# Reordering ScalarE's and VectorE's work in the last round before the final product, and moving one load ahead of stores

## The chip, the cores and the metric

The kernel runs on one core of one Trainium2 chip. The metric is the device time of one execution in microseconds (us); lower is better. Times shown beside each other come from runs of the same kernel on the same chip.

## What is computed

Attention with a window of 64 over 4 x 576 tokens and 8 heads of 64, then two feed-forward parts. Only the second one matters here:

```python
def _moe2_ref(x, w_in, w_out):          # x: 2304 x 512
    h = x @ w_in                        # 2304 x 2048
    g = np.maximum(0.01 * h, h)
    return (g @ w_out).astype(np.float32)
```

## The kernel before, in words

**Precision.** Every fp32 operand of a large product is split in two parts, hi (rounded to fp32r) and lo (the rest). ScalarE writes hi (an ACTIVATE Copy), VectorE then writes lo (a subtraction that reads hi). A product is three matmuls (`three_passes`, lines 387 to 391): hi x hi, hi x lo, lo x hi. Data are thus ready for TensorE only when VectorE's lo is written.

**Seven products for eight.** A block product is made by a Strassen-Winograd scheme: seven products P1 to P7 instead of eight, at the price of sums of the operands (g's sums here) and of the results (c11, c12, c21, c22). In the order of the code the products of a round are P1, P5, P6, P2, P7, P3, P4. ScalarE copies P1, P5 and P6 out of PSUM (`copy_p1`, `copy_p5`, `copy_u2`); VectorE adds P2, P7, P3 to them (`make_c11`, `make_c22`, `make_c12`).

**First product of the last part (x @ w_in).** 12 rounds, r = 15 to 26 (`h = r - HR0` = 0 to 11; HR = 12, OR0 = 27). A round is 14 half products of 6 matmuls of 128x384. After it ScalarE applies the leaky maximum in place: `leaky(r, 0)` to c11, `leaky(r, 2)` to c22, `leaky(r, 1)` to c12, and `leaky_c21` from PSUM. VectorE makes the sums of g: `g_sums13`, `g_sum2`, `g_sum4` for each of two halves s. SyncE stores the seven blocks of g to memory in four groups (`store_g(r, 0)` to `store_g(r, 3)`, of 1, 1, 3 and 2 DMAs of 384 KB each). The last round's g is not stored: it stays in SBUF and is used from there ("held").

**Second product (g @ w_out).** It runs over 84 parts k (`T_SEQ`), each of 12 matmuls. Each part of g is loaded back by `load_t(k)` on SyncE's queue (384 KB, DMA), unless held (k = 6, 7, 8, 12, ...), and split by `split_t(k)`, hi on ScalarE and lo on VectorE. `second_product(k)` waits for `t_lo >= k + 1`. The order of the first parts is P1's 0, 1, 2 (k = 0, 1, 2), P5's 0, 1, 2 (k = 3, 4, 5), then the held last parts of P1 and P5 (k = 6, 7), then P6 (k = 8 to 11). When part 6 is done, P1 is complete and `copy_p1(27)` may run; part 8 writes the same PSUM bank and waits for that copy (`bank_waits`, P6). On ScalarE `copy_p1(27)` stands behind `split_t(13)`, and so behind `split_t(11)` and `split_t(12)`.

**Buffers of the loads.** `t_raw` has 8 places. Parts 0 to 5, 9 and 10 take places 0 and 1 in turn; so `load_t(2)` waits for `t_lo >= 1`, `load_t(3)` for 2, `load_t(4)` for 3, `load_t(5)` for 4. Part 11 takes place 2 and part 13 place 3, which lie in g's own memory: they wait for the sums of g (`gt2_made >= 24`, all of `g_sum2`) and for `t_lo >= 8`. Places 4 and up wait for `g_sum4` too. Held parts wait for what makes them: part 6 for `leaky(26, 0)`, part 7 for both `g_sums13`, part 8 for both `g_sum2` (`t_ready`, lines 439 to 452).

**Units of w_out.** 8 units (fills f = 20 to 27) of weights are loaded by SyncE (`load_fill`: 384 and 512 KB) and split in two parts each by `split_fill(f, 0)` and `(f, 1)`. Part k = 2 needs units 24 and 25; part 6 needs 26 and 27. `load_fill(26)` waits until fill 24 is split (`fill_lo`), `load_fill(27)` until fill 25 is.

**What sets the order.** It is written out by hand: each engine executes its list in order, each wait holds what is behind it on that engine. In the last round (r = 26) before the change:

- ScalarE: split_t(0), copy_u2, fill 24, leaky 0, split_t(1), leaky 2, fill 25, split_t(2), leaky 1, leaky_c21, split_t(3), fill 26, split_t(4), fill 27, then split_t(5), (6), ...
- VectorE: split_t(0), c11, fill 24, c22, split_t(1), c12, fill 25, split_t(2), g_sums13 and g_sum2 of both halves, split_t(3), fill 26, split_t(4), fill 27, split_t(5), g_sum4, then split_t(6), (7), ...
- SyncE, from the end of round 25 on: store_g(25, 1), (25, 2), (25, 3), load_t(2), load_t(3), load_fill(26), load_t(4), load_fill(27), load_t(5), (9), (10), (11), ...

Of the kernel before, what the change touches and what calls it, by code (L numbers as in the profile page):

```python
# [35 lines left out]
NPROD = 7  # L36
# [5 lines left out]
HR0 = YR0 + NC2  # L42
# [119 lines left out]
TROUND = 4  # L162
# [46 lines left out]
def build(nc, qk_steps, v_steps, masks, w3, wo, w12, w_in, w_out, out):  # L209
    with ExitStack() as ctx:  # L210
# [262 lines left out]
        def _(sp):  # L473
# [224 lines left out]
            for r in range(HR0, OR0):  # L698
                h = r - HR0
                turn = h % ROUNDS == ROUNDS - 1 and h < HR - 1  # L700
                late = F_OUT + 2 * (h - HR + ROUNDS)
                if 2 <= h < 2 + NPAIR:
                    store_out_pre(h - 2)
                if h == 1:
                    for k in range(HRING):
                        load_hx(k)
                if h == 2 * ROUNDS - 3:
                    for k in range(NPROD, NPROD + HRING):
                        load_hx(k)
                if turn:  # L710
                    load_hx(NPROD * (h // ROUNDS) + HRING)
                if h == HR - 2:
                    load_t(0)
                if h == HR - 1:
                    load_t(2)
                    load_t(3)
                    load_fill(late)
                    load_t(4)
                    load_fill(late + 1)
                    continue  # L720
                if h > HR - ROUNDS:
                    load_fill(late)
                store_g(r, 0)
                if turn:
                    load_hx(NPROD * (h // ROUNDS) + HRING + 1)
                if 1 <= h <= NPAIR:
                    load_out_pre(h - 1)
                if h == HR - ROUNDS:
                    load_fill(late)
                if h == HR - 2:  # L730
                    load_t(1)
                if h >= HR - ROUNDS:
                    load_fill(late + 1)
                store_g(r, 1)
                if turn:
                    load_hx(NPROD * (h // ROUNDS) + HRING + 2)
                store_g(r, 2)
                store_g(r, 3)
            for k in range(5, TB):
# [57 lines left out]
        def _(act):  # L797
# [244 lines left out]
                if k >= NPROD and i == P3 and step == 0:  # L1042
                    store_y(c, P3, c22_done, 2 * r + 2)

            for r in range(HR0, OR0):
                h = r - HR0
                c = h // ROUNDS
                first, last = h % ROUNDS == 0 and h > 0, h % ROUNDS == ROUNDS - 1 and c + 1 < NC2
                late = F_OUT + 2 * (h - 1 - HR + ROUNDS)
                for s in range(2):  # L1050
                    copy_p1(r, s)
                if first:
                    split_hx(NPROD * (c - 1) + P3)
                if h in (1, 2):
                    split_fill(F_LATE + 2 * h - 1, 0)
                if h == 0:
                    store_y(NC2 - 1, P2, c21_done, 2 * HR0)
                    store_y(NC2 - 1, P6, t2_made, 2 * NC2)
                    store_y(NC2 - 1, P4, t4_made, 2 * NC2)
                for s in range(2):  # L1060
                    copy_p5(r, s)
                if h in (1, 2):
                    split_fill(F_LATE + 2 * h - 1, 1)
                if first:
                    split_hx(NPROD * (c - 1) + P4)
                if last:
                    split_hx(NPROD * c + P1)
                if h == HR - 1:
                    split_t(0)
                for s in range(2):  # L1070
                    copy_u2(r, s)
                if h == 0:
                    split_fill(F_LATE, 0)
                if h > HR - ROUNDS:
                    split_fill(late, 0)
                    split_fill(late, 1)
                leaky(r, 0, c11_done)
                if last:
                    split_hx(NPROD * c + P5)
                if h == HR - 1:  # L1080
                    split_t(1)
                if h == 0:
                    split_fill(F_LATE, 1)
                if h == 1:
                    split_fill(F_LATE + 2, 0)
                leaky(r, 2, c22_done)
                if h > HR - ROUNDS:
                    split_fill(late + 1, 0)
                    split_fill(late + 1, 1)
                if last:  # L1090
                    split_hx(NPROD * c + P6)
                if h == HR - 1:
                    split_t(2)
                if h == 1:
                    split_fill(F_LATE + 2, 1)
                leaky(r, 1, c12_done)
                if last:
                    split_hx(NPROD * c + P2)
                for s in range(2):
                    leaky_c21(r, s)  # L1100
                if last:
                    split_hx(NPROD * c + P7)
            for n in range(2):
                split_t(3 + n)
                for part in range(2):
                    split_fill(NFILL - 2 + n, part)

            for k in range(TROUND + 1, TB + NPROD):
                if k < TB:
                    split_t(k)  # L1110
                if k < NPROD:
                    continue
                c, i, _ = T_SEQ[k - NPROD]
                r, step = OR0 + c, T_STEP[k - NPROD]
                if step == JP - 1:
                    for s in range(2):
                        if i == P1:
                            copy_p1(r, s)
                        if i == P5:
                            copy_p5(r, s)  # L1120
                        if i == P6:
                            copy_u2(r, s)
                    if i == P4:
                        for s in range(2):
                            copy_c21(r, s)
                            if c == NC2 - 1:
                                store_last(s)
                if step == 1:
                    if i == P7:
                        store_out(c, 0, 0, c11_done)  # L1130
                    if i == P3:
                        store_out(c, 1, 1, c22_done)
                    if i == P4:
                        store_out(c, 0, 1, c12_done)
                    if i == P1 and c > 0:
                        store_out(c - 1, 1, 0, c21_done)
# [4 lines left out]
        def _(dve):  # L1141
# [263 lines left out]
            def split_t(k):  # L1405
                dve.wait_ge(t_hi, k + 1)
                t_ready(dve, k)
                hi, lo = [block_places[k % NPROD][:, n * BW:(n + 1) * BW].rearrange("p (j t) -> p j t", j=2) for n in range(2)]
                dve.tensor_tensor(lo, t_source(k), hi.bitcast(F32), ALU.subtract).then_inc(t_lo, 1)  # L1409
# [89 lines left out]
                    if i == P1 and step == 0 and c > 0:  # L1499
                        y_sum4(c - 1)  # L1500

            for r in range(HR0, OR0):
                h = r - HR0
                c = h // ROUNDS
                first, last = h % ROUNDS == 0 and h > 0, h % ROUNDS == ROUNDS - 1 and c + 1 < NC2
# [4 lines left out]
                    split_hx(NPROD * (c - 1) + P3)  # L1510
                if last:
                    split_hx(NPROD * c + P1)
                if h == HR - 1:
                    split_t(0)
                if 2 <= h < 2 + NPAIR:
                    out_sums(h - 2)
                for s in range(2):
# [20 lines left out]
                    split_fill(F_LATE + 2, 0)  # L1538
                if last:
                    split_hx(NPROD * c + P6)  # L1540
                if h == HR - 1:
                    split_t(1)
                for s in range(2):
                    make_c12(r, s)
                if h > HR - ROUNDS:
# [3 lines left out]
                    split_hx(NPROD * c + P2)  # L1549
                if h == 1:  # L1550
                    split_fill(F_LATE + 2, 1)
                if h == HR - 1:
                    split_t(2)
                g_sums13(r, 0)
                g_sum2(r, 0)
                g_sums13(r, 1)
                g_sum2(r, 1)
                if h in (0, 1):
                    fill_sums(F_LATE + 2 * h + 1)
                if h < HR - 1:  # L1560
                    for s in range(2):
                        g_sum4(r, s)
                if last:
                    split_hx(NPROD * c + P7)
            for n in range(2):
                split_t(3 + n)
                for part in range(2):
                    split_fill(NFILL - 2 + n, part)
            split_t(5)
            for s in range(2):  # L1570
                g_sum4(OR0 - 1, s)

            for k in range(TROUND + 2, TB + NPROD):
                if k < TB:
                    split_t(k)
                if k < NPROD:
                    continue
                c, i, _ = T_SEQ[k - NPROD]
                r, step = OR0 + c, T_STEP[k - NPROD]
                if step < JP - 1:  # L1580
                    continue
                for s in range(2):
                    if i == P2:
                        make_c11(r, s)
                    if i == P7:
                        make_c22(r, s)
                    if i == P3:
                        make_c12(r, s)
# [281 lines left out]
```

## Time and profile before

| | us |
|---|---|
| median of 3 runs | 755.67 |
| lowest and highest of them | 754.96 to 755.68 |
| the profiled execution's own time | 756.24 |
| its span, first to last instruction | 754.4 |
| TensorE busy (matmuls) | 741.9 |
| VectorE, ScalarE, GpSimd busy | 531.3, 420.4, 95.1 |
| DMA moved | 187.39 MB, mean 248 GB/s |

The span is what the trace shows; 1.8 us of the execution's time lie around it. Times in the rows are us from the start of the span. PE is TensorE's matmuls, PEld its weight loads, DVE is VectorE, ACT is ScalarE, SP SyncE and SPq its DMA issues. A matmul is listed with its full duration, and the next one starts before it ends.

### The profile page before, as it was taken

To read this page: it belongs to the slowest core of one execution; us is meant where nothing else is said; L and a number is where in the kernel's file an instruction comes from. 1 tells how busy PE (TensorE), PEld (TensorE's weight loads), DVE (VectorE), ACT (ScalarE), POOL (GpSimd) and SP (SyncE) were. 2 spreads that over 40 slices of the span, in tenths; PEclk is the share of its full clock that TensorE was granted. 3 is DMA by queue.
4 is the path that set the end of the run, shared out by engine and by line. 5 is a ranking of instruction groups with operands and counts; after the bars stand their busy time and mean duration, and the time that the engine had idled before them with its cause. 6 is when DMAs were issued, how large, how long until landed. Compare 5 with 4: busy or idle time off the path is not lost.

```text
span 754.4 us, 13228 instructions
## 1 busy us (share of the span) xinstructions
PE 741.9 (98%) x4744; PEld 715.7 (95%) x4744; DVE 531.3 (70%) x836; ACT 420.4 (56%) x901; POOL 95.1 (13%) x122
## 2 busy tenths in 40 slices
PE   8999999999999999999999999999998899999998
PEld 7887999999999999999999999999998899999998
DVE  5877998788656867888877968569689555455452
ACT  5866577545664445556556556456677544444441
POOL 2433374513343000000000000000000000000000
PEclk9999999999999999999999999999999999999999
DMA  9984677656874289988857987987997778778731
GB/s 332 304 301 150 234 242 227 223 157 219 276 233 142 98 260 337 329 274 315 285 192 296 330 296 273 347 299 252 365 373 266 232 211 224 220 206 237 210 105 63
DMA packets 97665, 187.39 MB, mean 248 GB/s; under 512 B 8000, under 2 KB 56256, under 8 KB 97600
## 3 DMA queue, kind: packets, MB, share of 16 engines
q1 hardware_dynamic: 91296, 173.57, 70.1%
q10 hardware_dynamic: 6304, 12.98, 4.5%
q8 instruction: 38, 0.62, 0.3%
q14 instruction: 27, 0.22, 0.1%
HBM read 117.31 MB, written 69.21 MB: 247 GB/s over the span
## 4 chain that ended last, share of the span: by engine, by line
PE 78%; DVE 8%; DMA 7%; issue 3%; ACT 2%; SPq 2%; POOL 0%; DVEq 0%; ACTq 0%
PE acc L389 14%; PE acc L391 14%; PE acc L390 13%; PE ps_scores L1616 4%; PE ps_more L389 3%; PE ps_more L391 3%; PE ps_more L390 3%; PE ps_values L1600 3%; PE ps_turned L1608 3%; DMA g_between<-arena 2%; PE ps_values L391 2%; PE ps_values L389 2%; PE ps_values L390 2%; PE ps_turned L391 2%; PE ps_scores L391 2%
## 5 line engine op out<-in xcount | busy, mean ns | idle before, releaser
L1409 DVE TENSOR_TENSOR parts<-arena,parts 128x768 fp32r<-128x768 f32 x72 | 68.6, 957 | 65.8 <-ACT parts L945 65.8
L389 PE MATMUL acc<-parts,weights_a 128*128 128x384 f32 (+1 forms) x296 | 103.6, 350 | 0.6 <-DVE arena L1345 0.5
L389 PE MATMUL acc<-parts,weights_b 128*128 128x384 f32 x296 | 100.8, 340 | 2.4 <-DVE parts L1409 2.4
L945 ACT ACTIVATE parts<-arena 128x768 fp32r<-128x768 f32 x72 | 60.7, 846 | 73.4 <-PE acc L391 36.5
L391 PE MATMUL acc<-parts,weights_a 128*128 128x384 f32 (+1 forms) x296 | 101.3, 342 | 0.0
L390 PE MATMUL acc<-parts,weights_a 128*128 128x384 f32 (+1 forms) x296 | 101.2, 342 | 0.0
L391 PE MATMUL acc<-parts,weights_b 128*128 128x384 f32 x296 | 99.5, 336 | 0.0
L390 PE MATMUL acc<-parts,weights_b 128*128 128x384 f32 x296 | 99.5, 336 | 0.0
L826 ACT ACTIVATE arena<-arena,negmax 128x128 f32<-128x128 f32 x144 | 56.0, 391 | 26.9 <-DVE negmax L1194 26.6
L389 PEld LDWEIGHTS acc<-parts,weights_a 128*128 128x128 f32 x296 | 55.6, 188 | 4.0 <-DVE arena L1345 1.0
L389 PEld LDWEIGHTS acc<-parts,weights_b 128*128 128x128 f32 x296 | 56.1, 190 | 3.0 <-DVE parts L1409 2.9
L921 ACT ACTIVATE arena<-arena 128x384 f32<-128x384 f32 x72 | 35.9, 524 | 40.6 <-DVE arena L1287 18.3
L391 PEld LDWEIGHTS acc<-parts,weights_a 128*128 128x128 f32 x296 | 55.6, 188 | 1.7
L390 PEld LDWEIGHTS acc<-parts,weights_a 128*128 128x128 f32 x296 | 55.7, 188 | 1.4
L390 PEld LDWEIGHTS acc<-parts,weights_b 128*128 128x128 f32 x296 | 56.1, 190 | 0.0
L391 PEld LDWEIGHTS acc<-parts,weights_b 128*128 128x128 f32 x296 | 56.0, 189 | 0.0
L896 ACT ACTIVATE parts<-arena 128x768 fp32r<-128x768 f32 x42 | 35.4, 848 | 32.2 <-PE ps_turned L391 11.7
L755 POOL TENSOR_TENSOR arena<-arena,rsum 128x512 f32<-128x512 f32 x36 | 37.4, 1040 | 124.1 <-DVE rsum L1202 124.1
L1355 DVE TENSOR_TENSOR parts<-arena,parts 128x768 fp32r<-128x768 f32 x42 | 39.6, 954 | 13.9 <-ACT parts L896 13.8
L1616 PE MATMUL ps_scores<-arena 128*128 128x128 f32 x288 | 38.3, 276 | 1.6 <-DMA arena<-qk_steps 1.5
L1616 PEld LDWEIGHTS ps_scores<-arena 128*128 128x128 f32 x288 | 35.2, 192 | 2.7 <-DMA arena<-qk_steps 2.2
L1189 DVE SCALAR_TENSOR_TENSOR arena<-ps_scores,arena 128x512 f32<-128x512 f32 x36 | 24.6, 684 | 12.8 <-PE ps_scores L1616 12.8
(236 smaller groups left out, 1880.1 us busy)
## 6 DMA issues: line engine op xcount, KB each, us to landing
g_between<-arena SPq DMA_DIRECT2D x77, 384.0 KB, 4.8
arena<-g_between SPq DMA_DIRECT2D x77, 384.0 KB, 3.6
arena<-qk_steps SPq DMA_DIRECT2D x36, 512.0 KB, 4.5
arena<-p_between SPq DMA_DIRECT2D x42, 384.0 KB, 5.0
arena<-v_steps SPq DMA_DIRECT2D x36, 256.0 KB, 3.3
p_between<-arena SPq DMA_DIRECT2D x24, 384.0 KB, 5.4
x_between<-arena ACTq DMA_DIRECT2D x21, 384.0 KB, 5.3
arena<-x_between SPq DMA_DIRECT2D x21, 384.0 KB, 5.3
```

Source lines behind the costliest of these rows:

```text
L389: eng.matmul(out_ap, w_hi, m_hi, start=start, stop=False, skip_group_check=resumed)
L390: eng.matmul(out_ap, w_hi, m_lo, start=False, stop=False, skip_group_check=resumed)
L391: return eng.matmul(out_ap, w_lo, m_hi, start=False, stop=stop, skip_group_check=resumed)
L755: pool.tensor_tensor(probs[:, r], probs[:, r], rsum[:, r * HP:(r + 1) * HP].unsqueeze(2).to_broadcast([P, HP, KW]), ALU.mult).then_inc(pro ...
L826: act.activation(probs[:, r, u], probs[:, r, u], ACT.Exp, bias=negmax[:, r * HP + u:r * HP + u + 1], scale=1.0, accum_out=sums[:, r * HP + ...
L896: act.activation(block_places[k % NPROD][:, 0:BW], ty_raw[TY_SLOT[k]], ACT.Copy).then_inc(ty_hi, 1)
L921: act.activation(g, g, ACT.Prelu, alpha=SLOPE).then_inc(g_done[q], 1)
L945: act.activation(block_places[k % NPROD][:, 0:BW].rearrange("p (j t) -> p j t", j=2), t_source(k), ACT.Copy).then_inc(t_hi, 1)
L1189: dve.scalar_tensor_tensor(out=probs[:, r], in0=ps_s[:, :].rearrange("p (h k) -> p h k", h=HP), scalar=float(D) ** -0.5, in1=picked.unsque ...
L1355: dve.tensor_tensor(b[:, BW:2 * BW], ty_raw[TY_SLOT[k]], b[:, 0:BW].bitcast(F32), ALU.subtract).then_inc(ty_lo, 1)
L1409: dve.tensor_tensor(lo, t_source(k), hi.bitcast(F32), ALU.subtract).then_inc(t_lo, 1)
L1616: last = pe.matmul(ps_s[:, w], qk[:, g % 2, w], qk[:, g % 2, DM + u * P:DM + (u + 1) * P], start=True, stop=True)
```

## The change

Nothing is added or removed: every instruction and every DMA is there before and after. The last round r = 26 is taken out of the loops of ScalarE and VectorE and gets lists of its own:

- ScalarE: split_t(0), copy_u2, split_t(1), fill 24, fill 25, leaky 0, leaky 2, split_t(2), split_t(3), leaky 1, leaky_c21, split_t(4), fill 26, split_t(5), fill 27, then split_t(6), (7), ...
- VectorE: split_t(0), c11, split_t(1), fill 24, c22, split_t(2), fill 25, split_t(3), c12, split_t(4), fill 26, split_t(5), fill 27, split_t(6), both g_sums13, split_t(7), both g_sum2, split_t(8), both g_sum4, then split_t(9), ...
- SyncE: `load_t(2)` goes from behind store_g(25, 3) to between store_g(25, 1) and store_g(25, 2).

```diff
@@ SyncE
                 if h == HR - 1:
-                    load_t(2)
                     load_t(3)
                     load_fill(late)
                     load_t(4)
...
                 store_g(r, 1)
                 if turn:
                     load_hx(NPROD * (h // ROUNDS) + HRING + 2)
+                if h == HR - 2:
+                    load_t(2)
                 store_g(r, 2)
                 store_g(r, 3)
@@ ScalarE
-            for r in range(HR0, OR0):
+            for r in range(HR0, OR0 - 1):
...
-            for n in range(2):
-                split_t(3 + n)
-                for part in range(2):
-                    split_fill(NFILL - 2 + n, part)
-
-            for k in range(TROUND + 1, TB + NPROD):
+            r = OR0 - 1
+            for s in range(2):
+                copy_p1(r, s)
+            for s in range(2):
+                copy_p5(r, s)
+            split_t(0)
+            for s in range(2):
+                copy_u2(r, s)
+            split_t(1)
+            for f in (NFILL - 4, NFILL - 3):
+                split_fill(f, 0)
+                split_fill(f, 1)
+            leaky(r, 0, c11_done)
+            leaky(r, 2, c22_done)
+            split_t(2)
+            split_t(3)
+            leaky(r, 1, c12_done)
+            for s in range(2):
+                leaky_c21(r, s)
+            for f in (NFILL - 2, NFILL - 1):
+                split_t(4 + f - NFILL + 2)
+                split_fill(f, 0)
+                split_fill(f, 1)
+
+            for k in range(TROUND + 2, TB + NPROD):
@@ VectorE
-            for r in range(HR0, OR0):
+            for r in range(HR0, OR0 - 1):
...
-            for n in range(2):
-                split_t(3 + n)
-                for part in range(2):
-                    split_fill(NFILL - 2 + n, part)
-            split_t(5)
+            r = OR0 - 1
+            split_t(0)
             for s in range(2):
-                g_sum4(OR0 - 1, s)
-
-            for k in range(TROUND + 2, TB + NPROD):
+                make_c11(r, s)
+            split_t(1)
+            split_fill(NFILL - 4, 0)
+            split_fill(NFILL - 4, 1)
+            for s in range(2):
+                make_c22(r, s)
+            split_t(2)
+            split_fill(NFILL - 3, 0)
+            split_fill(NFILL - 3, 1)
+            split_t(3)
+            for s in range(2):
+                make_c12(r, s)
+            for f in (NFILL - 2, NFILL - 1):
+                split_t(4 + f - NFILL + 2)
+                split_fill(f, 0)
+                split_fill(f, 1)
+            split_t(6)
+            g_sums13(r, 0)
+            g_sums13(r, 1)
+            split_t(7)
+            g_sum2(r, 0)
+            g_sum2(r, 1)
+            split_t(8)
+            g_sum4(r, 0)
+            g_sum4(r, 1)
+
+            for k in range(TROUND + 5, TB + NPROD):
```

## Rows read from the trace of the kernel before

**Rows 1.** The page: busy time of each engine.
```profile
PE 741.9 (98%) x4744; PEld 715.7 (95%) x4744; DVE 531.3 (70%) x836; ACT 420.4 (56%) x901; POOL 95.1 (13%) x122
```

**Rows 2.** Stretches: window, us, TensorE busy (matmuls), granted clock, DMA share, GB/s.
```profile
500.00:550.00 50.00, 49.99 (x288) 1.00 0.89 313
550.00:600.00 50.00, 45.22 (x247) 0.97 0.87 301
600.00:650.00 50.00, 50.00 (x290) 1.00 0.74 212
```

**Rows 3.** Timeline of TensorE, 569 to 592: first matmuls of parts 0 and 3 to 8.
```profile
569.02 0.33 PE L389 MATMUL acc<-parts,weights_a 128*128 128x384 f32 x1
...
577.05 0.44 PE L389 MATMUL ps_values<-parts,weights_a 128*128 128x384 f32 x1 [1.43 <-DVE parts L1409]
...
579.93 0.44 PE L389 MATMUL ps_values<-parts,weights_a 128*128 128x384 f32 x1 [0.49 <-DVE parts L1409]
...
582.80 0.44 PE L389 MATMUL ps_values<-parts,weights_b 128*128 128x384 f32 x1 [0.49 <-DVE parts L1409]
...
584.99 0.33 PE L389 MATMUL acc<-weights_a,weights_b 128*128 128x384 f32 x1
...
587.07 0.33 PE L389 MATMUL ps_values<-parts,weights_b 128*128 128x384 f32 x1
...
591.68 0.66 PE L389 MATMUL acc<-parts,weights_b 128*128 128x384 f32 x1 [2.37 <-DVE parts L1409]
```

**Rows 4.** Timeline of ScalarE, 571 to 592.
```profile
571.37 0.85 ACT L945 ACTIVATE parts<-arena 128x768 fp32r<-128x768 f32 x1 [2.58 <-DMA arena<-g_between]
572.13 0.92 ACT L921 ACTIVATE arena<-arena 128x384 f32<-128x384 f32 x2
...
573.69 0.84 ACT L945 ACTIVATE parts<-arena 128x768 fp32r<-128x768 f32 x1
...
588.85 1.58 ACT L945 ACTIVATE parts<-arena 128x768 fp32r<-128x768 f32 x2 [1.92 <-DMA arena<-g_between]
590.34 0.83 ACT L945 ACTIVATE weights_a<-arena 128x768 fp32r<-128x768 f32 x1
591.07 0.85 ACT L865 ACTIVATE arena<-acc 128x384 f32<-128x384 f32 x2
```

**Rows 5.** Timeline of VectorE, 561 to 588.
```profile
561.00 0.95 DVE L1409 TENSOR_TENSOR parts<-arena,parts 128x768 fp32r<-128x768 f32 x1
...
568.50 0.56 DVE L1307 TENSOR_TENSOR arena<-ps_values,arena 128x384 f32<-128x384 f32 x1 [1.08 <-DMA g_between<-arena]
...
574.59 0.95 DVE L1394 TENSOR_TENSOR arena<-arena 128x768 f32<-128x768 f32 x1
575.58 0.56 DVE L1398 TENSOR_TENSOR arena<-arena 128x384 f32<-128x384 f32 x1
576.05 0.95 DVE L1409 TENSOR_TENSOR parts<-arena,parts 128x768 fp32r<-128x768 f32 x1
576.92 2.08 DVE L1156 TENSOR_TENSOR weights_b<-arena,weights_b 128x768 fp32r<-128x768 f32 x2
...
584.47 3.55 DVE L1409 TENSOR_TENSOR parts<-arena,parts 128x768 fp32r<-128x768 f32 x4
```

**Rows 6.** Chain that ended last: start, us, what.
```profile
560.22 0.37 SPq L613
...
563.88 7.41 DMA arena<-g_between
...
585.50 3.27 DMA arena<-g_between
...
595.13 0.17 PE acc L390
```

**Rows 7.** DMA in a stretch, and the stores' (L613) time to landing, 500 to 620.
```profile
560.00:570.00 10.00, 10.00 (x59) 10.00 (x59) 8.44 (x14) 6.95 (x12) 0.00 (x0) 1.00 1.00 357
DMA to landing us min/median/max: 2.5/6.3/10.0
```

More of the change, by code:

```diff
@@ L1067, in _ @@
                     split_hx(NPROD * c + P1)
-                if h == HR - 1:
-                    split_t(0)
                 for s in range(2):
@@ L1079, in _ @@
                     split_hx(NPROD * c + P5)
-                if h == HR - 1:
-                    split_t(1)
                 if h == 0:
@@ L1091, in _ @@
                     split_hx(NPROD * c + P6)
-                if h == HR - 1:
-                    split_t(2)
                 if h == 1:
@@ L1512, in _ @@
                     split_hx(NPROD * c + P1)
-                if h == HR - 1:
-                    split_t(0)
                 if 2 <= h < 2 + NPAIR:
@@ L1540, in _ @@
                     split_hx(NPROD * c + P6)
-                if h == HR - 1:
-                    split_t(1)
                 for s in range(2):
@@ L1551, in _ @@
                     split_fill(F_LATE + 2, 1)
-                if h == HR - 1:
-                    split_t(2)
                 g_sums13(r, 0)
@@ L1559, in _ @@
                     fill_sums(F_LATE + 2 * h + 1)
-                if h < HR - 1:
-                    for s in range(2):
-                        g_sum4(r, s)
+                for s in range(2):
+                    g_sum4(r, s)
                 if last:
                     split_hx(NPROD * c + P7)
-            for n in range(2):
-                split_t(3 + n)
-                for part in range(2):
-                    split_fill(NFILL - 2 + n, part)
-            split_t(5)
-            for s in range(2):
-                g_sum4(OR0 - 1, s)
-            for k in range(TROUND + 2, TB + NPROD):
+            r = OR0 - 1
+            split_t(0)
+            for s in range(2):
+                make_c11(r, s)
[8 more added lines that the diff above has]
+            split_t(3)
+            for s in range(2):
+                make_c12(r, s)
[13 more added lines that the diff above has]
+            for k in range(TROUND + 5, TB + NPROD):
                 if k < TB:
```

## The prediction

> **What bounds the kernel now.** First the busy times on the page: TensorE is busy for 741.9 of 754.4 us [rows 1], so a reorder on other engines can give back only its idle time. The table of stretches shows where that is: 50 of 50 us are busy on either side, but only 45.22 between 550 and 600, and that is the only stretch of the three with a granted clock under 1.00 [rows 2]. This is where the first product goes over into the second. TensorE's timeline shows the parts of the second product there [rows 3]. Part 7 starts 2.08 us after part 6: that is a part without a wait. Part 0 starts at 569.02, so part 8 would start at 569.02 + 8 x 2.08 = 585.7. It starts at 591.68, 6.0 us late: about 1.8 us are lost ahead of part 3, 0.8 each ahead of parts 4 and 5, 2.5 ahead of part 8. Behind it the clock is at half: eleven matmuls take 595.13 - 591.68 = 3.45 us in place of 11 x 0.173 = 1.9, another 1.5 us [rows 3, 6].
>
> Two different chains make this loss. Parts 3 to 5 wait for VectorE's splits: load_t(2) lands at 571.3 (issued 563.88, 7.41 us behind five stores) [rows 6], ScalarE splits part 2 at 571.37 [rows 4], and VectorE reaches split 3 at 576.05 only after four sums of g, the last two of which stand in [rows 5]. Part 8 is put down to VectorE's split, but the one it needs, of part 8, was the second of four run in a row from 584.47 on, and long done [rows 5]. What ended at 591.5 is copy_p1(27) on ScalarE, which part 8's bank waits for: it starts at 591.07, right behind the splits of parts 11, 12 and 13, and those had waited for load_t(11), issued at 585.50 and landed 3.27 us later [rows 4, 6]. load_t(11) needs split 7 and all of g_sum2. **Part 8 is the last wait of the passage; from there on TensorE runs without a gap. So the change is worth what it does to the start of part 8, whatever parts 3 to 5 gain.**
>
> **The change, part by part.** Nothing is added, so only starts move. Steps used: a split on ScalarE 0.85 us, the next instruction 0.74 later; a split on VectorE 0.95, the next 0.87 later; both parts of a fill 2.08 on VectorE, 2.0 with the overlap into the next instruction; g_sums13 0.95, the next 0.87 later when it need not wait for it; g_sum2 0.56, the next 0.48 later; a pair of leaky 0.92 [rows 4, 5].
>
> *load_t(2) ahead of the stores.* It waits for VectorE's split 0, which ends at 561.95 [rows 5]; so it goes out at 562.0, not 563.88. It now has none of the five stores ahead, and lands at about 566 (3.27 us alone [rows 6], more behind what is still queued). The stores pay: store_g(25, 2) began at 560.22 and now begins at 562.4, behind the load. Its landing sets c12 of round 26, which started at 568.50 on that landing [rows 5]; I put the new one at 568.4 + 2.2 = 570.6, and at 564 + 10.0 = 574.0 if its last DMA, issued near 564, were as slow as the slowest store of the region [rows 7]. In the new order c12 comes up on VectorE at 574.1, so this costs nothing; if the cover went, each us behind 574.1 would be a us of the chain below. load_t(3) gains nothing: the same five stores and load_t(2) are ahead of it in the one queue as before, and the queue is full (357 GB/s, DMA share 1.00 [rows 7]). 384 KB at that rate are 1.1 us, so it lands near 571.3 + 1.0 = 572.3 in both kernels (bounds: 571.3, with load_t(2), and 573.7, when ScalarE of before took it with no wait for a DMA [rows 4]).
>
> *Splits 2 and 3 early, sums late.* ScalarE: split 1, fills 24 and 25 and the two leaky pairs are done by 568; split 2 at 568, VectorE 0.9 later, fill 25 done at 571.8, ahead of part 2 at 573.2. Split 3 starts with its landing: ScalarE 572.3 to 573.15, VectorE 573.2 to 574.15. Part 3 can start at 569.02 + 3 x 2.08 = 575.3, so its wait is gone: a gain of 1.75 us there.
>
> *From there VectorE is the chain.* c12 at 574.1 and 574.55. ScalarE's leaky 1 follows it to 575.6, leaky_c21 takes 0.74 more, then split 4 at 576.3; VectorE's split 4 is 577.2 to 578.15. Part 4 starts 578.2 (it was 579.93). Fill 26 to 580.1, split 5 to 581.05: part 5 at 581.1 (582.80). Fill 27 to 582.95, split 6 to 583.9: part 6 at 584.0 (584.99). Up to here the change is ahead by 1.0 us, and the lead has shrunk at each step. Then come the sums: both g_sums13, 583.8 to 585.65. Split 7 needs them, on ScalarE too: ScalarE 585.7 to 586.55, VectorE 586.6 to 587.55, with VectorE idle for 0.9 us meanwhile. Part 7 at 587.6 (587.07): now behind. Both g_sum2: 587.45 to 588.5. **load_t(11) waits for them and goes out at 588.55 in place of 585.50.** It lands at 588.55 + 3.27 = 591.8; ScalarE's splits 11, 12, 13 take 3 x 0.74 = 2.2, the first half of copy_p1 0.47: 594.5. Part 8 starts at 594.6 in place of 591.68: **+2.9 us**. TensorE's waits ahead of parts 4 to 8 are 0.8, 0.8, 0.8, 1.5 and 4.9 us: 8.9 with roundings, against 6.0.
>
> Of this sum the DMA's 3.27 is the one term with a page beside it. The Trainium skill ("DMA: Bandwidth & Descriptors", Anatomy of one DMA) gives, for another issue path, a fixed 2.0 us and the bytes at 436 GB/s. For 393 kB that is an estimate of 2.9 us; by it the sum would be +2.5. I take the row, as it is this load itself.
>
> *g_sum4 last.* It now ends near 592 instead of 583.6. load_t(18) and (19) wait for it, but part 18 is due 10 parts, some 21 us, behind part 8: hidden.
>
> *The clock.* Before, TensorE idled 2.37 us ahead of part 8, and the clock fell for 3.45 us, at a cost of 1.5 us. Now the wait is 4.9 us. I take the same fall plus a little: +0.3. Bounds: it does not fall at all (-1.5), or stays low as long again (+1.7).
>
> Sum: +2.9 + 0.3 = +3.2 us. Against the profiled execution's 756.24 that is 759.4 (span 757.6). That execution is 0.57 above the median, so against the median of the runs, 755.67, it is 758.9.
>
> **The rivals.**
>
> *Forecast, 0.70:* the chain through the late sums, load_t(11) and copy_p1; about 758.9, on its own 757.2 to 760.5.
>
> *The clock stays low, 0.15.* With 4.9 us of idling and four shorter waits ahead of it, the low clock may last twice as long once part 8 runs: +1.7, and 760.6 to 761.5. For it: the one gap of over 2 us in the stretch is the one with a fall. Against: three short waits ahead of it brought none. The Trainium skill ("TensorE: Matmul & The Clock Gate", What's actually happening) says that the default state is throttled and activity releases it; a longer idle time can by this only keep or lengthen the fall.
>
> *The gain survives and it is faster, 0.06.* The one mechanism is the load queue. If load_t(3), now with load_t(2) long gone, were served early, at 569.5 and not 572.3, split 3 would start behind fill 25 at 571.6, and VectorE's chain would run 1 to 2 us earlier. The point that decides is g_sum2's end: load_t(11) must be out before 585.50, that is 3.0 us sooner than worked out. VectorE's own work from split 3 to the end of g_sum2 is 12 us (four more splits, two fills, c12, the sums) and starts no earlier than 571.6; with the hand-overs to ScalarE, 585.5 is hardly reached. With 2.0 us from the early landing, VectorE's 0.9 us of idling ahead of split 7 gone and no fall of the clock: 2.9 - 2.0 - 0.9 - 1.5 = -1.5, so 754.2.
>
> *It comes out even, 0.09.* The early landing takes 1.5 off, and a shorter fall of the clock 1 more: 3.2 - 2.5 = +0.7, so 756.4.
>
> *The stores are the new wait* (part of the forecast's upper end): store_g(25, 2) and (25, 3) held behind load_t(2), which needs split 0. It decides from a landing behind 574.1, 3.5 us later than worked out, and would add at most 1 us.
>
> **How the numbers follow.** A measurement of this kernel tells some 0.2% (1.5 us) from no change. Slower by more than that: the forecast, the clock, in all 0.85. Faster 0.06, within 0.09. The range takes in the clock's low end and half of the even case, and the long fall: 756.8 to 761.6.
>
> **What the profile would show.** Right: no wait ahead of part 3 (start near 575.3 counted from part 0 at 569.0), waits of 0.5 to 1 us ahead of parts 4, 5 and 6, a longer one ahead of 7, and nearly 5 us ahead of part 8; load_t(2) issued before the stores' line; load_t(11) issued some 19.5 us behind part 0 instead of 16.5; ScalarE's split 11 waiting for a DMA, copy_p1 directly ahead of TensorE's restart. Outside 550 to 600 all stretches equal. Wrong: part 8 within 22.5 us of part 0's start, or load_t(11) ahead of g_sum2's end, or c12 waiting for a store at 574.

## The result and the profile after

The changed kernel takes 759.66 us (median of 6 runs, 758.82 to 760.53), the kernel before 755.67 beside it. The ratio is 1.0057, 95% interval 1.0044 to 1.0070: slower by 4.0 us, where 758.9 was forecast. The two kernels measured again later (run r1_changed) gave 759.72 against 755.85, ratio 1.0049 [1.0032, 1.0066].

The loss is in the one stretch. Stretches of the changed kernel (columns: window, us, TensorE, weight loads, VectorE, ScalarE, GpSimd busy, clock, DMA share, GB/s):

```profile
500.00:550.00 50.00, 50.00 (x288) 49.47 (x287) 38.84 (x65) 30.44 (x58) 0.00 (x0) 1.00 0.89 317
550.00:600.00 50.00, 42.25 (x224) 40.54 (x223) 36.45 (x48) 31.44 (x50) 0.00 (x0) 0.93 0.79 276
600.00:650.00 50.00, 50.00 (x290) 50.00 (x289) 25.81 (x30) 22.63 (x30) 0.00 (x0) 1.00 0.75 211
```

Against [rows 2] the neighbours are equal and the middle one has lost 3.0 us of busy TensorE, with the clock at 0.93 in place of 0.97. The profiled execution of the changed kernel is its quickest (758.82), and in it part 0 starts at 567.74, against 569.02 (569.07 in the trace of r1_changed, 759.81 us). So the way to part 0 took 1.3 us less in one execution of this kernel than in another, and the parts are best compared by their distance from part 0. TensorE's timeline of the changed kernel:

```profile
567.74 0.33 PE L389 MATMUL acc<-parts,weights_a 128*128 128x384 f32 x1
...
576.95 0.45 PE L389 MATMUL ps_values<-parts,weights_a 128*128 128x384 f32 x1 [0.72 <-DVE parts L1423]
...
579.82 0.44 PE L389 MATMUL ps_values<-parts,weights_b 128*128 128x384 f32 x1 [0.52 <-DVE parts L1423]
...
582.69 0.44 PE L389 MATMUL acc<-weights_a,weights_b 128*128 128x384 f32 x1 [0.51 <-DVE weights_a L1423]
...
586.36 0.45 PE L389 MATMUL ps_values<-parts,weights_b 128*128 128x384 f32 x1 [1.29 <-DVE parts L1423]
...
593.43 0.66 PE L389 MATMUL acc<-parts,weights_b 128*128 128x384 f32 x1 [4.72 <-ACT arena L866]
```

No wait stands ahead of part 3 now. Parts 4, 5, 6, 7 and 8 start 9.2, 12.1, 15.0, 18.6 and 25.7 us behind part 0; before [rows 3] it was 10.9, 13.8, 16.0, 18.1 and 22.7. The lead of 1.7 us at part 4 is gone by part 7, and part 8 is 3.0 us late. This time the releaser that the profile names, ScalarE's copy (L866), is the true one, as experiment 3 will show. Behind it the clock is at half, as the chain that ended last shows:

```profile
594.09 0.32 PE acc L390
...
598.54 0.17 PE acc L389
```

Sixteen matmuls take 598.54 - 593.43 = 5.1 us, from start to start, where 16 x 0.173 = 2.8 would do: 2.3 us lost, against 1.5 for eleven before.

What ScalarE did ahead of that copy:

```profile
579.89 0.83 ACT L946 ACTIVATE weights_a<-arena 128x768 fp32r<-128x768 f32 x1
584.47 0.84 ACT L946 ACTIVATE parts<-arena 128x768 fp32r<-128x768 f32 x1 [3.74 <-DVE arena L1408]
587.33 2.31 ACT L946 ACTIVATE parts<-arena 128x768 fp32r<-128x768 f32 x3 [2.02 <-DVE arena L1412]
590.60 1.58 ACT L946 ACTIVATE parts<-arena 128x768 fp32r<-128x768 f32 x2 [0.96 <-DMA arena<-g_between]
592.09 0.83 ACT L946 ACTIVATE weights_a<-arena 128x768 fp32r<-128x768 f32 x1
592.82 0.85 ACT L866 ACTIVATE arena<-acc 128x384 f32<-128x384 f32 x2
```

Splits 6, 7, then 8 to 10, then 11 and 12, 13, and the copy. ScalarE stands idle 3.74 us for the two g_sums13 (L1408) and 2.02 us for g_sum2 (L1412), then 0.96 us for load_t(11). VectorE in the same time, and the chain that ended last:

```profile
581.68 0.95 DVE L1423 TENSOR_TENSOR weights_a<-arena,weights_a 128x768 fp32r<-128x768 f32 x1
582.55 1.82 DVE L1408 TENSOR_TENSOR arena<-arena 128x768 f32<-128x768 f32 x2
585.34 0.96 DVE L1423 TENSOR_TENSOR parts<-arena,parts 128x768 fp32r<-128x768 f32 x1 [0.97 <-ACT parts L946]
586.22 1.02 DVE L1412 TENSOR_TENSOR arena<-arena 128x384 f32<-128x384 f32 x2
```

```profile
587.30 3.22 DMA arena<-g_between
...
592.91 0.38 ACT arena L866
593.30 0.14 issue
593.43 0.66 PE acc L389
```

load_t(11) goes out 0.06 us after g_sum2, 19.6 us behind part 0, where it was 16.5 before [rows 6], and lands in 3.22. The chain goes on over the copy to part 8.

### The profile page after: what moved, and what is told of

Its sections match the earlier page's. It is cut to its first block, busy times and chain, and to the rows that moved or that the text cites. A ratio compares the mean times of both kernels' runs of the same rounds, so it can differ in the third digit from the quotient of the medians.

```text
span 757.0 us, 13228 instructions
## 1 busy us (share of the span) xinstructions
PE 742.8 (98%) x4744; PEld 716.5 (95%) x4744; DVE 531.3 (70%) x836; ACT 420.5 (56%) x901; POOL 95.7 (13%) x122
## 4 chain that ended last, share of the span: by engine, by line
PE 74%; DMA 9%; DVE 8%; ACT 3%; issue 3%; SPq 2%; POOL 1%; DVEq 0%; ACTq 0%
PE acc L389 13%; PE acc L391 13%; PE acc L390 13%; PE ps_scores L1644 3%; PE ps_more L389 3%; PE ps_more L391 3%; PE ps_more L390 3%; PE ps_values L1628 2%; PE ps_turned L1636 2%; PE ps_values L389 2%; PE ps_values L391 2%; PE ps_values L390 2%; DMA g_between<-arena 2%; PE ps_scores L389 2%; PE ps_turned L389 2%
## 5 line engine op out<-in xcount | busy, mean ns | idle before, releaser
L1369 DVE TENSOR_TENSOR parts<-arena,parts 128x768 fp32r<-128x768 f32 x42 | 39.7, 954 | 13.8 <-ACT parts L897 13.7
```

The lines of the kernel that those rows point to most:

```text
L1369: dve.tensor_tensor(b[:, BW:2 * BW], ty_raw[TY_SLOT[k]], b[:, 0:BW].bitcast(F32), ALU.subtract).then_inc(ty_lo, 1)
```

## The experiments

All ratios are to the kernel before, measured beside each of them. D8 is the start of part 8 behind part 0 in the one profiled execution: 22.7 before, 25.7 after. Between the two traces of one kernel D8 differs by up to 1.1 us (0.4 for the changed kernel), so a small step needs more than D8 to show it.

**1. Only the load moved.** The kernel before with `load_t(2)` ahead of store_g(25, 2).

> The kernel before with only load_t(2) moved ahead of store_g(25, 2). Theory (late sums of g and load_t(11) make the loss): no change, 755.7 within 0.5 us; part 8 starts 22.7 us behind part 0, as before, because load_t(3) lands no earlier. Rival (the stores held behind the load make the loss): slower, 757 to 760, with c12 of round 26 waiting for a store by more than 1.1 us and part 3 no earlier.

Measured: 756.26 us against 755.95, ratio 1.0003 [0.9991, 1.0014]; D8 23.6. With the old lists the move is worth nothing. It does what was said of the stores: c12 waits longer for them, 2.06 us against 1.08 [rows 5], in VectorE's timeline of this run:

```profile
569.26 0.56 DVE L1308 TENSOR_TENSOR arena<-ps_values,arena 128x384 f32<-128x384 f32 x1 [2.06 <-DMA g_between<-arena]
```

That start is 1.0 us behind part 0, where the prediction had put it at 1.6 (570.6 - 569.02). D8 is 0.9 later than expected: split 2 stands behind c12 and fill 25 here, and parts 2 and 3 start 0.7 us later. How much of it comes from the move is open: in experiment 6, with the load in its old place, parts 2 and 3 are 0.5 us late too.

**2. Only the lists.** The changed kernel with `load_t(2)` back behind the stores.

> The changed kernel with load_t(2) back behind the stores: only the two lists are new. Theory: slower than the changed kernel, as load_t(2) lands at 571 and holds split 2 and all behind it on VectorE: part 8 starts 27.5 us behind part 0 (25.7 in the changed kernel), about 761.5 us. Rival (the held stores are the cost): faster than the changed kernel, 756 to 758.

Measured: 761.85 us, ratio 1.0075 [1.0057, 1.0092]; D8 27.0. So the new lists alone make the kernel slower. With these lists, where nothing on ScalarE or VectorE may pass split 2, the early load gives back 2.2 us by the medians and 1.4 by the ratios (0.0018 x 756), and 1.3 in the traces' D8; in the traces VectorE's split 3 starts 5.3 us behind part 0 in place of 4.2. The intervals of the two ratios overlap, so that the load gives back something rests on the medians and on the traces. The loss is in the lists.

**3. The copy freed.** On ScalarE of the changed kernel:

```diff
             for k in range(TROUND + 2, TB + NPROD):
+                if k == 11:
+                    for s in range(2):
+                        copy_p1(OR0, s)
                 if k < TB:
                     split_t(k)
...
-                if step == JP - 1:
+                if step == JP - 1 and k != 13:
```

> The changed kernel with ScalarE's copy_p1(27) moved from behind split 13 to ahead of split 11. Theory (part 8 waits for this copy, and the copy for load_t(11)): part 8 starts 21.6 us behind part 0 in place of 25.7, the clock falls less or not at all: 4.1 + 1 to 2.5 us off 759.7, that is 753.1 to 754.6. Rival (part 8 waits for VectorE's late sums and splits themselves): part 8 no more than 1 us earlier, 758.5 or more.

Measured: 754.33 us, ratio 0.9979 [0.9970, 0.9988]; D8 22.3, 0.7 later than worked out; no matmul of part 8 at half clock. ScalarE and TensorE in this run:

```profile
588.12 2.31 ACT L946 ACTIVATE parts<-arena 128x768 fp32r<-128x768 f32 x3 [2.02 <-DVE arena L1415]
590.33 0.85 ACT L866 ACTIVATE arena<-acc 128x384 f32<-128x384 f32 x2
```

```profile
590.95 0.41 PE L389 MATMUL acc<-parts,weights_b 128*128 128x384 f32 x1 [1.45 <-ACT arena L866]
```

The copy is now behind splits 8 to 10 only. One instruction pair, moved past three splits, takes 5.3 us off (3.4 in D8; the other 1.9 go with the fall of the clock, which is gone; 5.1 in the repeats of both kernels beside each other), and the changed kernel becomes quicker than the one before. The repeat was expected thus:

> The changed kernel with copy_p1(27) ahead of split 11 again: 753.5 to 755, part 8 21.6 to 22.3 behind part 0.

It gave 754.62, ratio 0.9981 [0.9967, 0.9995], D8 23.1, that is 0.8 above the upper end of what was expected: all its parts from 4 on are late by that much. From part 7 to part 8 it is 3.8 us in both traces, against 7.1 and 7.2 in the two of the changed kernel.

**4. g_sum2 ahead of split 7.** On VectorE of the changed kernel:

```diff
             g_sums13(r, 1)
-            split_t(7)
             g_sum2(r, 0)
             g_sum2(r, 1)
+            split_t(7)
             split_t(8)
```

> The changed kernel with both g_sum2 ahead of VectorE's split 7. Theory: gt2_made comes 1.0 us earlier, so load_t(11), copy_p1 and part 8 do too: part 8 24.7 us behind part 0, 758.7 us. Rival (the sums do not matter, only the copy's queue or the clock): part 8 unchanged at 25.7, 759.7.

Measured: D8 24.7, as worked out; 759.26 us, ratio 1.0037 [1.0024, 1.0049]. The trace shows the step: from part 7 to part 8 it is 6.3 us, against 7.1 and 7.2. Its way is a little other than expected. g_sum2 now runs where VectorE had stood idle for 0.97 us ahead of split 7, and ends 2.1 us sooner (17.4 behind part 0 in place of 19.5); load_t(11) then waits for the end of split 7, and goes out at 18.5, 1.1 sooner. The time does not tell it from the changed kernel: 0.4 us by the medians, 1.5 by the ratios, with intervals that overlap.

**5. TensorE kept busy in the wait.** In the changed kernel, ahead of part 8; the results are read by nobody, and the output stays as it was:

```diff
+                if k == 8:
+                    pe.wait_ge(c21_done, 2 * OR0)
+                    for _ in range(24):
+                        pe.matmul(ps_s[:, 0:CT], units[0][:, 0, 0:P], units[0][:, 0, P:P + CT], start=True, stop=True)
                 second_product(k)
```

> The changed kernel with 24 matmuls of 128x384, whose result nobody reads, put on TensorE between parts 7 and 8 (4.2 us, inside its wait of 4.9). Theory for the rest of the loss (behind the wait the clock runs at half, which costs 1 to 2.5 us): part 8 still starts 25.7 us behind part 0, no matmul of it at half clock, 757.2 to 758.7 us. Rival (the wait is the whole loss): 759.7, or 760 where the added matmuls end later than the copy.

Measured: 758.42 us, ratio 1.0039 [1.0024, 1.0054]. The time is in the range expected and no matmul of part 8 is at half clock, but D8 is 26.4, 0.7 later than expected, and the interval overlaps that of the change. So it was repeated beside the changed kernel itself.

> The changed kernel again, as the base for the next three on one chip. Every theory: 759 to 760 us, ratio to the kernel before 1.004 to 1.007, part 8 25.7 us behind part 0 within 0.7.

> The changed kernel with the 24 idle-time matmuls again. If the fall of the clock costs 1 us or more in the changed kernel, this is 1 to 2 us under the changed kernel of this call, though part 8 starts no earlier. If the clock costs nothing, it is equal or slower.

Changed kernel: 759.72 (758.73 to 760.26), D8 26.1. With the added matmuls: 757.77 (756.49 to 758.38), ratio 1.0024 [1.0012, 1.0036], D8 26.5. No run of one lies among those of the other, so 1.95 us came from matmuls that nobody reads, though part 8 started 0.4 us later. The stretch of the changed kernel, then with the added matmuls (window, us, TensorE busy, clock, DMA share, GB/s):

```profile
550.00:600.00 50.00, 41.83 (x226) 0.97 0.79 276
```

```profile
550.00:600.00 50.00, 45.72 (x257) 1.00 0.80 276
```

The clock stays at 1.00 in the second. This agrees with the Trainium skill ("TensorE: Matmul & The Clock Gate", What's actually happening), by which activity releases the throttle.

**6. The copy freed in the kernel before.** The edit of experiment 3 on the old lists.

> The kernel before with copy_p1(27) ahead of split 11. Theory (the copy's place behind load_t(11) was a loss of the kernel before too): part 8 starts 19.3 to 19.9 us behind part 0 in place of 22.7 and the clock does not fall: 4.3 us off 755.9, 751 to 752.5. Rival (part 8 waited for VectorE's split, as the profile of before has it): part 8 at 22.7, 755.9.

Measured: 751.84 us, ratio 0.9950 [0.9935, 0.9965]. D8 is 20.8, about 1 later than worked out (small waits ahead of parts 2 and 5), but there is no wait ahead of part 8 and no fall of the clock. ScalarE and TensorE in this run:

```profile
586.38 0.85 ACT L945 ACTIVATE parts<-arena 128x768 fp32r<-128x768 f32 x1 [1.82 <-DMA arena<-g_between]
587.13 0.90 ACT L865 ACTIVATE arena<-acc 128x384 f32<-128x384 f32 x2
589.25 1.58 ACT L945 ACTIVATE parts<-arena 128x768 fp32r<-128x768 f32 x2 [1.22 <-DMA arena<-g_between]
```

```profile
589.42 0.33 PE L389 MATMUL acc<-parts,weights_b 128*128 128x384 f32 x1
```

The copy stands behind split 10 now, and split 11 still waits for its load (1.22 us), but part 8 starts without it. So the profile's releaser for part 8 of the kernel before, VectorE's L1409 [rows 3], was the wrong one: nothing on VectorE was changed here.

**7. Both edits on the changed kernel.**

> The changed kernel with both edits, g_sum2 ahead of split 7 and copy_p1(27) ahead of split 11. Theory: the two gains are of one chain and add only as far as it is the last wait: part 8 starts 20.0 to 20.7 us behind part 0 (22.3 with the copy alone), 752 to 753 us. Rival (g_sum2's place matters through load_t(11) alone, so with the copy freed it gives nothing): part 8 at 22.3, 754.3.

Measured: 753.03 us, ratio 0.9966 [0.9954, 0.9978], D8 22.1: later than worked out, in an execution whose part 5 started 1.2 us later than worked out (13.3 behind part 0). That did not tell the two theories apart, so it was repeated next to the repeat of experiment 3.

> The changed kernel with both edits again. If g_sum2's place matters beyond load_t(11), since split 8 needs it too: 1 to 1.6 us under the copy alone, part 8 right behind part 7 with no wait. If it acts through load_t(11) alone: equal to the copy alone.

752.83 us, ratio 0.9958 [0.9943, 0.9972], D8 21.0, no wait ahead of part 8; 1.8 us under the copy alone. g_sum2's place counts beyond load_t(11): split 8 needs it as well, and the freed copy stands behind split 8. The medians and the waits ahead of part 8 say this (1.43 us with the copy alone, none in both traces with both edits); the two intervals of the ratios still overlap.

**8. A version that beats both.** load_t(2) stays ahead of the stores. ScalarE: as changed up to leaky 2, then split 2, leaky 1, split 3, leaky_c21, split 4, fill 26, splits 5 and 6, fill 27, splits 7 and 8, copy_p1, splits 9 on. VectorE:

```diff
             split_fill(NFILL - 3, 1)
-            split_t(3)
             for s in range(2):
                 make_c12(r, s)
-            for f in (NFILL - 2, NFILL - 1):
-                split_t(4 + f - NFILL + 2)
-                split_fill(f, 0)
-                split_fill(f, 1)
-            split_t(6)
+            split_t(3)
             g_sums13(r, 0)
             g_sums13(r, 1)
-            split_t(7)
             g_sum2(r, 0)
             g_sum2(r, 1)
-            split_t(8)
+            split_t(4)
+            split_fill(NFILL - 2, 0)
+            split_fill(NFILL - 2, 1)
+            split_t(5)
+            split_t(6)
+            split_fill(NFILL - 1, 0)
+            split_fill(NFILL - 1, 1)
+            split_t(7)
+            split_t(8)
```

> The changed kernel with c12, all g_sums13 and all g_sum2 before split 4, split 6 ahead of fill 27, and copy_p1(27) ahead of split 9. Theory: with the sums early and the copy freed, parts 5 to 8 run without a wait of their own: part 3 at 6.3, part 4 at 9.6, part 8 at 18.7 us behind part 0, 750 to 751 us. Rival (early sums only push the splits of parts 3 to 5 back by as much): part 8 at 21 or later, 753 or more.

Measured: 750.47 us, ratio 0.9934 [0.9918, 0.9950]; part 3 without a wait, part 4 at 9.4, D8 18.6. TensorE's timeline of this run has two waits left in the passage, and part 8 follows part 7 at once:

```profile
578.39 0.45 PE L389 MATMUL ps_values<-parts,weights_a 128*128 128x384 f32 x1 [0.91 <-DVE parts L1429]
...
581.27 0.44 PE L389 MATMUL ps_values<-parts,weights_b 128*128 128x384 f32 x1 [0.49 <-DVE parts L1429]
...
587.62 0.33 PE L389 MATMUL acc<-parts,weights_b 128*128 128x384 f32 x1
```

The early sums cost part 4 nothing against the changed kernel (9.4, and 9.2 to 9.5 in its two traces). In the changed kernel VectorE stood idle for 2.08 us ahead of split 4:

```profile
575.93 0.96 DVE L1423 TENSOR_TENSOR parts<-arena,parts 128x768 fp32r<-128x768 f32 x1 [2.08 <-ACT parts L946]
```

Here the sums, 2.7 us from their start to the start of split 4, fill that place, and split 4 follows them with no wait:

```profile
574.71 1.82 DVE L1414 TENSOR_TENSOR arena<-arena 128x768 f32<-128x768 f32 x2
576.45 1.02 DVE L1418 TENSOR_TENSOR arena<-arena 128x384 f32<-128x384 f32 x2
577.39 0.95 DVE L1429 TENSOR_TENSOR parts<-arena,parts 128x768 fp32r<-128x768 f32 x1
```

This version holds several edits at once. Experiments 3, 4 and 7 show what the places of the copy and of g_sum2 are worth in the changed kernel; what c12, g_sums13 and split 6 add was not run singly.

## Why the prediction was right

**What bounds the kernel.** Right: only the passage counts, and in it the start of part 8. Experiment 6 shows that this holds for the kernel before too, against the releaser that its profile names. All runs together bear it out. Taking D8 off the median time leaves 731.0 to 732.0 us in the eight runs whose trace has no fall of the clock behind part 7 (experiments 3 and 5 to 8 with their repeats), and 732.7 to 734.8 us in the six with one (before, after, its second measurement, experiments 1, 2 and 4). The runs come from more than one chip; the medians of the kernel before beside them lie within 0.5 us.

**load_t(2) and the stores.** Right in sign and place. It went out at 560.41, 7.33 us ahead of part 0 (7.0 worked out), and c12 of round 26, at 572.83, waited for no store: the cover held. load_t(3) went out at 565.41; ScalarE's split 3 began at 571.08 on its landing, 3.34 us behind part 0, where 3.3 was worked out (572.3 - 569.02):

```profile
571.08 0.85 ACT L946 ACTIVATE parts<-arena 128x768 fp32r<-128x768 f32 x1 [3.68 <-DMA arena<-g_between]
572.83 0.55 DVE L1321 TENSOR_TENSOR arena<-ps_values,arena 128x384 f32<-128x384 f32 x1
```

The whole chain was anchored on that landing. The reason given, that the load gains nothing from the move because the bytes ahead of it in the queue are the same, is not shown: ScalarE of the kernel before did not wait for this load, so its landing there cannot be read. What the move is worth was left unpriced by itself: nothing with the old lists, 1.3 to 2.2 us with the new.

**The chain on VectorE.** Every start was worked out from durations of the kernel before. In distances from part 0:

| start of | worked out | measured |
|---|---|---|
| part 4 | 9.2 | 9.2 |
| part 5 | 12.1 | 12.1 |
| part 6 | 15.0 | 15.0 |
| part 7 | 18.6 | 18.6 |
| load_t(11) | 19.5 | 19.6 |
| part 8 | 25.6 | 25.7 |

The price of the 3.27 us for load_t(11) held (3.22); the estimate of 2.9 us worked out from the Trainium skill ("DMA: Bandwidth & Descriptors", Anatomy of one DMA), which is for another issue path, would have put part 8 at 25.2.

**The clock** is the term that was mis-sized. +0.3 us was taken. Of the 4.0 us measured, 3.0 are the later start of part 8, so about 1.0 is left; the two traces give 2.3 - 1.5 = 0.8 for the clock. In the second trace of the changed kernel the fall is no longer than before (1.6 us lost), but part 8 starts 3.4 us later in place of 3.0. So one pair of traces does not fix how the last 1 us is shared.

The prediction also took for granted that the kernel before always pays its 1.5 us. The mean granted clock of each whole execution says otherwise. (The traces without a fall show 0.999 or 1.000.) In 25 of the 70 executions of the kernel before that were measured beside the experiments it is 1.000, in the others 0.997 or 0.998 (0.998 in the traced one, with its fall of 3.45 us), and those are slower by 1.0 to 1.5 us in their medians. The 12 executions of the changed kernel lie at 0.995 to 0.998, none at 1.000. So the fall seems to come in every execution now, where it came in some two thirds of them before; this part of the loss is not in the prediction. Experiment 5 puts the full cost of the fall in the changed kernel at about 2 us (1.95 by the medians; 2.3 and 1.6 in the two traces). The rival of a clock that stays low as long again (+1.7) did not come about in full. Its time was added up wrongly, too: 760.6 is the forecast plus 1.7 and so counts the forecast's +0.3 beside it; 2.9 + 1.7 on 755.67 is 760.3.

**The other rivals.** The faster case asked for load_t(3) at 569.5, 0.5 us behind part 0; it came at 3.3, 2.8 us later. The even case needed the same. The stores as the new wait were hidden in the change, and cost nothing measurable with the old lists (experiment 1).

## What to carry to other kernels

Where several buffers pass from one stage to the next, find the last wait of the passage, and the whole chain to it, before giving the early ones a better order: here the first parts came 1.7 us sooner, and the sums that pay for it held back a load, three splits and a copy, in that order. On an engine that executes its list in order, try a small copy that frees a PSUM bank ahead of the instructions that wait for a transfer; here moving one pair of copies was worth 3.6 us in the one kernel and 5.3 in the other, more than any other single edit tried. Where a wait needs several semaphores, find for each the instruction that it really needs and when that one ended. In the kernel before the profile named VectorE, whose split of part 8 had long been done; the copy was the last.

## What was not expected

The clock may fall after TensorE has taken up work again. In experiment 4 part 8 starts at 593.32 behind a wait of 3.95 us, runs six matmuls 0.18 apart, and only then goes to 0.32 (their listed time goes from 0.34 to 0.52):

```profile
593.32 0.41 PE L389 MATMUL acc<-parts,weights_b 128*128 128x384 f32 x1 [3.95 <-DVE parts L1423]
593.57 0.34 PE L390 MATMUL acc<-parts,weights_b 128*128 128x384 f32 x1
593.75 0.35 PE L391 MATMUL acc<-parts,weights_b 128*128 128x384 f32 x1
593.93 0.34 PE L389 MATMUL acc<-parts,weights_b 128*128 128x384 f32 x1
594.11 0.34 PE L390 MATMUL acc<-parts,weights_b 128*128 128x384 f32 x1
594.29 0.33 PE L391 MATMUL acc<-parts,weights_b 128*128 128x384 f32 x1
594.46 0.46 PE L389 MATMUL acc<-parts,weights_b 128*128 128x384 f32 x1
594.72 0.52 PE L390 MATMUL acc<-parts,weights_b 128*128 128x384 f32 x1
```

The trace of experiment 1 shows the same: six matmuls at full speed behind a wait of 2.54 us, then the fall. In the traces a wait of 1.45 us (experiment 3) was followed by no fall, those of 2.4 and more (before, after, experiments 1, 2 and 4) all were. What lies between was not tried, and the wait alone does not settle it: of the executions of the kernel before, one in three shows no fall in its mean clock. The clock's cost behind equal waits varied too: in the first trace of the changed kernel the stretch had a clock of 0.93, in the second 0.97, with waits of 4.72 and 4.80 us.
